# Attention with a top-k mask and a gated product: TensorE's parts of a slot in another order

## The reference

```python
# q, k, v: (4, 8, 576, 64) float32
scores = scale * np.matmul(q, k.transpose(0, 1, 3, 2))
kth = np.partition(scores, -32, axis=-1)[..., -32:-31]
scores = np.where(scores >= kth, scores, -1e9)
attn = np.exp(scores - np.max(scores, axis=-1, keepdims=True))
attn = attn / (np.sum(attn, axis=-1, keepdims=True) + 1e-09)
attn_out = np.matmul(attn, v)
x = attn_out.transpose(0, 2, 1, 3).reshape(2304, 512)
a = x @ w_a                  # (512, 1536)
b = x @ w_b                  # (512, 1536)
out = (a * b) @ w_out        # (1536, 512)
```

## Time and profile before

| | |
|---|---|
| median of 3 runs | 810.61 us (809.99 to 811.42) |
| the profiled execution | 810.42 us |
| its span | 808.3 us |
| TensorE busy | 769.5 us (95%), weight loads 688.5 us (85%) |
| VectorE busy | 738.6 us (91%) |
| ScalarE busy | 663.5 us (82%) |
| GpSimd busy | 505.4 us (63%) |

### The profile page before, as it was taken

The page is one execution under the profiler, slowest core; times in us unless marked ns, Lnnn a source line. Parts: engine busy times, 40 slices in busy tenths (PEclk is TensorE's granted clock), DMA queues, the critical chain, the costliest instruction groups (busy, mean ns, idle before and its releaser), DMA issues.

```text
span 808.3 us, 18438 instructions
## 1 busy us (share of the span) xinstructions
PE 769.5 (95%) x5952; PEld 688.5 (85%) x5952; DVE 738.6 (91%) x1593; ACT 663.5 (82%) x1624; POOL 505.4 (63%) x560
## 2 busy tenths in 40 slices
PE   5458899999999999999999999999999999999998
PEld 4347789899989898998888889889998888888887
DVE  7999999998999999999999999999999999999500
ACT  5888988888788888888888888888788888888732
POOL 3999976666555666666655666666655565655532
PEclk9967999999999999999999999999999999999999
DMA  6655864435644344445644443443563434343562
GB/s 183 169 165 166 290 196 136 139 103 152 177 144 139 125 137 140 142 137 147 181 130 144 116 142 116 140 139 110 145 177 124 137 125 137 125 135 118 170 215 86
DMA packets 117246, 119.17 MB, mean 147 GB/s; under 512 B 61856, under 2 KB 80288, under 8 KB 117152
## 3 DMA queue, kind: packets, MB, share of 16 engines
q1 hardware_dynamic: 116880, 117.93, 48.3%
q10 hardware_dynamic: 272, 0.07, 0.0%
HBM read 108.53 MB, written 9.44 MB: 146 GB/s over the span
## 4 chain that ended last, share of the span: by engine, by line
PE 89%; DVE 5%; POOL 2%; issue 2%; ACT 1%; DMA 1%; SPq 0%; POOLq 0%; ACTq 0%
PE ps L586 38%; PE ps L618 19%; PE ps L555 10%; PE ps L521 9%; PE ps L537 8%; PE ps L597 3%; DVE best L978 2%; DVE work L995 2%; PE ps L490 1%; DMA stage<-in_w 1%; PE ps L499 1%; POOL w_lo L857 1%; POOL scores L902 1%; POOL k_t L857 0%; DMA k_rows<-in_k 0%
## 5 line engine op out<-in xcount | busy, mean ns | idle before, releaser
L978 DVE MAX8 best<-work 128x8 f32<-128x576 f32 x432 | 308.4, 766 | 0.0
L902 POOL TENSOR_TENSOR scores<-scores,keep 128x576 f32<-128x576 f32 x144 | 205.6, 1432 | 36.6 <-ACT keep L713 36.1
L995 DVE MATCH_REPLACE8 work<-best,work 128x576 f32<-128x576 f32 x288 | 214.9, 766 | 0.0
L586 PE MATMUL ps<-w_hi,x_hi 128*128 128x384 f32 x576 | 202.7, 352 | 2.0 <-issue 1.1
L586 PE MATMUL ps<-w_hi,x_lo 128*128 128x384 f32 x576 | 194.6, 338 | 0.0
L909 POOL TENSOR_TENSOR ab<-ab 128x384 f32<-128x384 f32 x72 | 73.3, 1018 | 166.0 <-ACT ab L771 166.0
L586 PE MATMUL ps<-w_lo,x_hi 128*128 128x384 f32 x432 | 146.1, 338 | 0.0
L745 ACT COPY probs_t<-ps 128x512 f32<-128x512 f32 x144 | 81.8, 587 | 50.7 <-PE ps L537 49.8
L586 PEld LDWEIGHTS ps<-w_hi,x_hi 128*128 128x128 f32 x576 | 108.4, 188 | 16.7 <-issue 13.7
L722 ACT ACTIVATE scores<-scores,neg 128x576 f32<-128x576 f32 x144 | 114.2, 820 | 2.2 <-POOL scores L902 1.9
L737 ACT ACTIVATE scores<-scores,inverse 128x576 f32<-128x576 f32 x144 | 115.9, 806 | 0.1
(11 more groups left out here) (64 smaller groups left out, 1312.7 us busy)
## 6 DMA issues: line engine op xcount, KB each, us to landing
wo_lo<-x_scratch SPq DMA_DIRECT2D x69, 768.0 KB, 4.5
wb_lo<-x_scratch SPq DMA_DIRECT2D x70, 384.0 KB, 4.1
stage<-in_w SPq DMA_DIRECT2D x36, 256.0 KB, 3.0
x_scratch<-k_t SPq DMA_DIRECT2D x18, 256.0 KB, 2.6
k_rows<-in_k SPq DMA_DIRECT2D x32, 128.0 KB, 4.7
v_rows<-in_v SPq DMA_DIRECT2D x32, 128.0 KB, 2.6
out<-stage SPq DMA_DIRECT2D x16, 256.0 KB, 4.1
q_rows<-in_q SPq DMA_DIRECT2D x63, 64.0 KB, 3.6
```

The lines of the kernel that those rows point to most:

```text
L586: last = mm(ps_ab[which], x[:, g % 2, kb, :], w, start=(kb == 0 and m == 0), stop=(kb == KB - 1 and m == 2))
L902: V.tensor_tensor(row, row, keep[:, j, :], ALU.add).then_inc(mask_done, 1)
L978: ins = V.max(best[:, u % 2, j, 8 * r:8 * r + 8], src)
L995: V.match_replace(out=work[:, j, :], in_to_replace=best[:, u % 2, j, 8 * r:8 * r + 8], in_values=src, imm_value=NEG).then_inc(chain, 1)
```

## The change

`late_blocks(n)` returns all four blocks of a for steps 0 to 67, that is for slots 5 to 72. So in these slots nothing of a is computed ahead of the turns, and all of it stands behind `q_transposes`, next to b. ScalarE's program asks the same function: in these slots the copy of a stands in the next slot, behind the exponentials. Output moves from behind `q_transposes` to right behind the scores, in all slots up to 73. The last slots are as before. Instructions, buffers and semaphores stay the same.

```diff
         def late_blocks(n):
 
 
+            if 0 <= n <= NU - MOE0:
+                return (0, 1, 2, 3)
             if not 0 <= n < NCH or n % NH:
                 return ()
             return (2, 3) if UNITS[PER * (n // NH)][1] == FULL else (3,)
...
                 probs_v(s - 2)
                 qk(s + 1)
-                if s == NU + 1:
+                if s <= NU + 1:
                     output(n - 2)
                 columns_of(n, 0, (0, 1, 2, 3)[:4 - len(late_blocks(n))])
-                if s == NU:
-                    output(n - 2)
                 wait(pe, xraw_done, min(s - 1, NU))
                 turn_hidden(n - 1)
                 transposes(s - 1, 0)
...
                 q_transposes(s + 3)
-                if s < NU:
-                    output(n - 2)
                 columns_of(n, 0, late_blocks(n))
                 columns_of(n, 1, (0, 1, 2, 3))
```

## The result

The changed kernel takes 813.29 us in the median of 12 runs (812.38 to 817.55), the kernel before 810.85 us beside it on the same chip (12 runs, 809.95 to 811.89). The ratio is 1.0037, with an interval of 1.0028 to 1.0046. So it is slower, by 2.4 us in the medians and by 3 us in the ratio; the most likely case of the prediction was no change at 811.8 us. The profiled execution took 812.75 us, its span is 810.6 us, 2.3 us more than the span before.

The account below looks back on a forecast made before the run. It took TensorE, busy without gaps, to bound the kernel. Slots 21 and 57 -1.0, fourteen later slots -0.1, start +2.1 and end +0.3 summed to +1.3 us, so 811.8 us, range 809.3 to 813.6.

Parts of the forecast that it names:

- Bound and steady slots: TensorE is busy without gaps, so steady slots change by nothing, between -0.03 and +0.03 us each.
- a boundary less: Rival: a and b form one run of matmuls, saving 0.1 us in 63 slots, 6 us, to 805.6; chance 0.08.
- both move by the same distance, so about 8 us stay: Slot 38: output and its wo_lo transfer's issue, at the previous output's end, shift equally, keeping about 8 us for landing.
- if output waits in slots behind 9: Sign that the prediction is wrong: output waiting in any slot later than 9.
- Slots 21 and 57: Where only half of a stood ahead of the turns, output there lets transposes meet finished weights: -0.5 us each, -1.0.
- The end: Slot 72: turns behind output alone wait 2.1 us for the product, other waits go: +0.3 us, bounds 0 to +0.6.
- The start: Slots 5 to 8: output in slot 8 waits 2.1 us for its wo_lo transfer, and 2.1 us stay.
- Only some 0.1 should pass on: Argument against the spreading start: ScalarE had other work until then, so only some 0.1 us of slip reaches the issue.
- So that is hidden: Slot 5: the part behind the turns grows by 1.6 us, hidden because slot 6's transposes wait for ScalarE until 82.50.
- The transfer is hidden anyway: Rival: slot 8's transfer lands in 4.5 us or less, the start costs 0.3 to 0.5, total 810.0; chance 0.17.
- The start spreads: Rival: slot 6's later b delays copies, product, stores and the transfer's issue by 1 us, total 812.8; chance 0.13.
- The clock falls: Rival: idle stretches of 2.1 us in slots 8 and 72 lower the clock, costing 1.7 us, total 813.5; chance 0.15.

Follow-up runs that it names:

- e3: Changed kernel with a put back ahead of the turns in slots 5 to 9, output still early: 815.40 us, ratio 1.0056.
- e4: Changed kernel with the wo_lo transfers for the outputs of slots 7 and 8 issued first in SP's slot, not last: 812.68 us, ratio 1.0030.
- The four pairs above: Four pairs of kernels differing only in slot 72; with a ahead of the turns, time was lower by 1.8, 0.9 and 0.6 us, and higher by 0.5.
- e6: Kernel before with only a moved behind the turns in slots 5 and 6, output unmoved: 812.27 us, ratio 1.0025.
- e9: e6 plus unread filling matmuls where a had stood, nine in slot 5 and twelve in slot 6: 809.70 us, ratio 0.9993.
- e8: Changed kernel with all of a ahead of the turns again in slot 72, between output and the turns: 813.48 us, ratio 1.0043.
- e13: Changed kernel with filling matmuls in slots 5 and 6 and a ahead of the turns in slot 72, transfers not early: 812.40 us, ratio 1.0019.
- e10: Changed kernel plus unread filling matmuls, nine in slot 5 and twelve in slot 6: 812.84 us, ratio 1.0030.
- all three together: Changed kernel with filling matmuls (slots 5, 6), early transfers (slots 7, 8) and a ahead of the turns in slot 72: 809.98 us, ratio 0.9993.
- look_a: Changed kernel unaltered, executed and profiled again to look for falls of the clock: 817.01 us.
- e1: Changed kernel with the old order in slots 2 to 9, new order from slot 10 on: 810.57 us, ratio 0.9999.
- e12: Changed kernel with slots 5 and 6 as before as to a, the rest changed: 812.41 us, ratio 1.0027.

## Why the prediction went wrong

- **Bound and steady slots: right but for slots 20 and 56.** TensorE sets the time of slots 10 to 71, whatever the order. Slot 38 takes 10.15 us. The rival "a boundary less" asked for 6 us and is false: nothing came. In slot 38 the slacks held: the low part 2.3 us (2.6 foretold), ScalarE's copy inside its idle time. The argument "both move by the same distance, so about 8 us stay" holds in that slot; in slots 20 and 56 the issue doesn't move with the output before it, and output is 0.1 to 0.7 us late in half of the profiles. That is the prediction's own sign of being wrong, "if output waits in slots behind 9", though small. The prediction went by the starts of the matmuls, where the Trainium skill (Perfetto Trace Analysis, Identifying the Most-Contended Engine) judges TensorE's headroom by MFU, the share of the peak arithmetic rate, and by weight-load time. No run here shows the MFU. Of the tenth of headroom that the prediction read from the weight loads this change gained nothing: no matmul of a steady slot moved closer to the next.
- **Slots 21 and 57: right.** 0.55 us each, 0.5 foretold. The fourteen quarter slots and the rest gave 0.3 us together, 0.1 foretold.
- **The end: right in size.** 0.3 us and a wait of 1.93 us (2.1 foretold). What it left out is the clock, except as a rival: this wait of 1.9 us is in eight profiles, and behind it the clock fell in two, e3 and e4, for 3.4 us; there slot 72 takes 1.9 us more than before. The four pairs above give 0.5 us of loss to 1.8 us of gain for avoiding it.
- **The start: wrong, +3.15 for +2.1** (+2.64, if the 0.51 ahead of slot 5 is left out). This is the step that failed, and in these places.
  - *The first transfer was left out of the sum.* The prediction let slot 7 run as 2.23, 2.19, 1.34 and 4.4 and looked for the wait only in slot 8. Output of slot 7 had moved 3.6 us forward too. It would start at 88.1 plus 2.23, 90.3; its transfer had landed at 90.8 in the kernel before, and with the 6.2 us of the earlier trace rows in place of its own 5.2 it would land at 91.8. That is 0.5 to 1.5 us of wait, one slot earlier. It measured 2.28, and slot 8's 0.34 instead of 2.1.
  - *The start spread.* "Only some 0.1 should pass on" was held against this rival, for slot 8's transfer. Slot 7's was issued 1.12 us later, because slot 6 starts later and with it the copies and GpSimd's product, and slot 8's at 97.23 and not at 96.37, beyond the rival's bound of 96.8. That it makes only 0.34 us of wait is because slot 7 had already lost the time.
  - *The clock of slots 5 and 6 wasn't asked about.* "So that is hidden" held for the queue: slot 7 starts 0.8 us late by the change, as foretold. But TensorE stands still where a had been, and what runs at 1.2 GHz behind it grows: by 0.35 us of cost in the changed kernel's profile and by 1.2 in e6's slot 5. e6 loses 2.0 us so, and e9 none of it. The prediction read the earlier trace rows, the fall in these very slots, and asked only whether a new wait would bring one, not whether moving work out of an old wait would prolong one.
- **Rivals.** "The transfer is hidden anyway" is false: slot 8's took 6.2 us again. (Its sum was also added wrongly: with 0.3 to 0.5 for the start it is -0.5 to -0.3 and not -0.6.) "The start spreads" is partly true, as above. "The clock falls", at 813.5 with 0.15, is nearest to the time measured, and its sign that decides, a clock of 0.50 behind 98 us, isn't in the profile of the first result; it is in one of the two later executions of the same kernel and in e3, e4 and e8, and in e13 a clock of 0.50 ends at 96.7. That its number is nearest is in part luck: the profile without such a fall took 812.75 us, and its loss at the start comes from slot 7's transfer. But its chance was too low: it counted the waits of 1.2 us that brought no fall as evidence for waits of 2 us and more.
- **Sum.** From the profile it is +3.15 for the start, +0.2 for slot 20, -1.1 for slots 21 and 57, -0.3 for the slots around them and +0.35 for the end: +2.3 on the span, where +1.3 was foretold. The error is the start's 1.05, of which 0.5 arose ahead of slot 5. The time lies in the range, but above 812.2, on the side to which 0.35 was given; 0.55 stood on no change.

**The repairs do not add.** One repair alone moves little (by the ratios e4 0.6 us less, e10 0.6 less, e8 0.5 more, none of them clear of the uncertainty), all three together 3.6, which is. What the filling gives in slots 5 and 6 is taken by the wait for the transfer, which ends when that lands; and what the transfer gives was lost again in slot 72 in e4's profile.

**Left open.** How often the clock falls. Of nine profiles in which slot 7's output waits 1.5 us or more, it fell in four: e3, e8 and look_a with the three longest waits (2.81, 3.30, 3.87 us; the fall begins within them) and e13 (1.99 us), and not in five (1.54, 1.85, 1.92, 2.27, 2.28 us). Why one transfer takes 5.4 us in one execution and 7.8 in another of the same kernel was not tested either. That e1 has before's median while its profile is 0.8 us shorter, and that e12's median lies above its profile, would fit falls or long transfers in part of the executions; it was not shown.

## What to carry to other kernels

On an engine without gaps an order of parts is worth nothing in itself; read only the slots in which it waits, and there hold each moved part against every input it needs, from the first slot on, with that transfer's own row, and in the slots whose queue carries extra loads as well. Work that stands in an idle place at the start of a pipeline can keep the clock up, so count what its removal does to the granted clock before calling it hidden. When one engine's part is put back, put back the other engine's matching copy too, or leave a part between, and repair all the causes at once and take them away singly: here no single repair showed what it was worth. Where executions differ by 4 us, as here, a profile of one shows a mechanism and not its size in the median.

## What the runs showed of the hardware that was not expected

- 21 additional matmuls of 384 columns, whose product nobody reads, made a kernel 2.6 us faster by the ratios (1.0025 to 0.9993), as the granted clock went from 0.50 to 1.00 in the stretch from 70.6 to 77.3 us. The Trainium skill (TensorE: Matmul & The Clock Gate, Part 1) says that "the default state is throttled, and activity releases the throttle". By that, matmuls in an idle place keep the clock up, and e9 agrees: 0.50 without them, 1.00 with them.
- The same program met nearly the same idle place (1.59 and 1.76 us busy of 3.30) and in one execution ran 6.8 us at 1.2 GHz from there on, in the other none; 817.01 and 813.19 us.
- The same transfer of 768 KB, issued at 87.4 and 87.3 us in two executions of the same program, took 7.8 and 5.4 us to land; the median of these transfers in the changed kernel's profile is 4.6 us.
